# Ordering twelve scatters behind a gather, and moving three row squares out of the last attention head

## The reference

```python
x = attn_out.transpose(0, 2, 1, 3).reshape(1536, 512)
xn = x / (np.linalg.norm(x, axis=-1, keepdims=True) + 1e-06)
logits = xn @ en.T / tau
expert_idx = np.argmax(logits, axis=1)
gate_w = softmax(logits)[token, expert_idx]
for e in range(8):
    mask = expert_idx == e
    h = np.maximum(x[mask] @ w1[e], 0.0)
    out[mask] = gate_w[mask, None] * (h @ w2[e])
```

## Time and profile before

| | |
|---|---|
| median of 3 runs | 775.69 us (775.42 to 775.87) |
| the profiled execution | 775.23 us |
| its span, first to last instruction | 773.4 us |
| PE busy | 748.8 us, 97% of the span |
| DVE, ACT, POOL busy | 607.8, 462.3, 372.5 us |
| mean granted clock of TensorE | 0.986 of full speed |

### The profile page before, as it was taken

The page is one execution under the profiler, slowest core; times in us unless marked ns, Lnnn a source line. Parts: engine busy times, 40 slices in busy tenths (PEclk is TensorE's granted clock), DMA queues, the critical chain, the costliest instruction groups (busy, mean ns, idle before and its releaser), DMA issues.

```text
span 773.4 us, 15683 instructions
## 1 busy us (share of the span) xinstructions
PE 748.8 (97%) x5369; PEld 696.1 (90%) x5372; DVE 607.8 (79%) x1011; ACT 462.3 (60%) x887; POOL 372.5 (48%) x346
## 2 busy tenths in 40 slices
PE   7899999999999978999999999999999999999996
PEld 4799999999999956999999999989899999999995
DVE  5788888888888988766677765899977777778774
ACT  4778887788887872222222222468776767667673
POOL 3767767776566207664234442947332323223232
PEclk9999999999999986999999999999999999999999
DMA  9411112111140058467544676600000000000000
GB/s 265 110 33 32 42 31 51 31 31 41 31 153 1 1 191 295 113 238 243 202 158 158 229 245 202 236 1 1 1 28 1 28 1 28 0 0 27 0 27 27
DMA packets 70147, 68.27 MB, mean 88 GB/s; under 512 B 31704, under 2 KB 55128, under 8 KB 70112
## 3 DMA queue, kind: packets, MB, share of 16 engines
q1 hardware_dynamic: 67104, 60.31, 24.8%
q0 software_dynamic: 2080, 7.29, 2.5%
q10 hardware_dynamic: 928, 0.23, 0.1%
HBM read 56.99 MB, written 10.83 MB: 88 GB/s over the span
## 4 chain that ended last, share of the span: by engine, by line
PE 58%; issue 22%; POOL 8%; DVE 7%; ACT 3%; DMA 1%; POOLq 0%; ACTq 0%; DVEq 0%
PE PS L556 8%; PE PS L558 8%; PE PS L557 8%; PE PS L430 8%; POOL HL L1005 6%; PE PS L404 4%; PE PS L405 4%; PE PS L389 4%; PE PS L390 4%; PE PS L371 3%; PE PS L413 2%; POOL out L1014 1%; PE PS L363 1%; PE PS L552 1%; DVE w_low L1128 1%
## 5 line engine op out<-in xcount | busy, mean ns | idle before, releaser
L556 PE MATMUL PS<-XH,w_high 128*128 128x256 f32 x640 | 182.4, 285 | 0.7 <-DVE XL L1298 0.6
L558 PE MATMUL PS<-XH,w_low 128*128 128x256 f32 x640 | 182.1, 285 | 0.0
L557 PE MATMUL PS<-XL,w_high 128*128 128x256 f32 x640 | 182.1, 285 | 0.0
L906 POOL TENSOR_SCALAR w_high<-w_raw 128x1024 fp32r<-128x1024 f32 x80 | 102.6, 1300 | 97.1 <-DMA w_raw<-in_moe_w 82.0
L1005 POOL TENSOR_TENSOR HL<-U,HH 128x512 fp32r<-128x512 f32 x48 | 63.1, 1314 | 173.7 <-ACT HH L842 173.7
L556 PEld LDWEIGHTS PS<-XH,w_high 128*128 128x128 f32 x640 | 123.8, 194 | 4.0 <-issue 2.2
L557 PEld LDWEIGHTS PS<-XL,w_high 128*128 128x128 f32 x640 | 123.8, 193 | 1.7
L558 PEld LDWEIGHTS PS<-XH,w_low 128*128 128x128 f32 x640 | 123.8, 193 | 0.0
L1144 DVE TENSOR_TENSOR PTL<-PS,PTH 128x384 fp32r<-128x384 f32 x192 | 98.0, 552 | 32.0 <-ACT PTH L727 31.6
L1128 DVE TENSOR_TENSOR w_low<-w_raw,w_high 128x1024 fp32r<-128x1024 f32 x77 | 114.4, 1513 | 1.3 <-issue 1.2
L727 ACT ACTIVATE PTH<-PS 128x384 fp32r<-128x384 f32 x192 | 83.7, 489 | 42.5 <-PE PS L430 41.9
(11 more groups left out here) (209 smaller groups left out, 1670.4 us busy)
## 6 DMA issues: line engine op xcount, KB each, us to landing
w_raw<-in_moe_w SPq DMA_DIRECT2D x64, 512.0 KB, 7.4
xs<-xs_dram SPq DMA_DIRECT2D x8, 578.0 KB, 3.9
w_raw<-in_moe_w_in SPq DMA_DIRECT2D x8, 512.0 KB, 8.2
w_raw<-in_moe_w_out SPq DMA_DIRECT2D x8, 512.0 KB, 6.2
QK<-in_q SPq DMA_DIRECT2D x16, 192.0 KB, 3.1
V<-in_v SPq DMA_DIRECT2D x16, 192.0 KB, 2.4
QK<-in_k SPq DMA_DIRECT2D x15, 192.0 KB, 3.2
x_dram<-XO SPq DMA_DIRECT2D x1, 1728.0 KB, 7.2
```

The source lines that it names most:

```text
L556: nc.tensor.matmul(o, wh, xh, start=first, stop=False)
L557: nc.tensor.matmul(o, wh, xl, start=False, stop=False)
L558: return nc.tensor.matmul(o, wl, xh, start=False, stop=last)
L906: return nc.gpsimd.tensor_scalar(HIGH[par][:, p, :], RAW[par][:, p, :], 1.0, 0.0, ALU.mult, ALU.add)
```

## The change

The order of three squares on ACT changes, and POOL waits once more. In the last head the squares of tiles 3 and 4 (steps 1 and 2) are taken out; behind the head ACT now does tile 3, the first copy of `OS`, tile 4, the second copy, tile 5. Before, tile 5 was squared ahead of both copies. On POOL the first scatter waits for the landing of the second gather too.

```diff
-                        if far and i < GT:
-                            square(2 + i)
+                        if far and i == 0:
+                            square(2)
...
-            square(JT - 1)
+            square(JT - 3)
             for n, t0, t1 in ((0, 0, GT - 1), (1, GT - 1, GT)):
...
                 act.wait_ge(pv_done, GROUPS + n)
                 nc.scalar.activation(OS[:, t0 * P:t1 * P], PS[:, n, 0:(t1 - t0) * P], ACT.Copy).then_inc(os_done, 1)
+                square(JT - 2 + n)
             act.wait_ge(last_part, 1)
             act.wait_ge(xo_done, GROUPS)
...
             pool.wait_ge(scaled, 1)
+            pool.wait_ge(first_in[1], 16)
             for t in range(NT):
                 nc.gpsimd.indirect_dma_start(xs_dram, bass.IndirectOffsetOnAxis(ap=pos_i[:, t:t + 1], axis=0), XO[:, t, :], None).then_inc(rows_sent, 16)
```

## The result

The changed kernel takes 781.35 us, median of 4 runs (779.97 to 781.67); the kernel before took 775.56 us beside it (4 runs, 773.83 to 775.87). The ratio is 1.0068, with a 95% interval of 1.0057 to 1.008: 0.7% slower. The profiled execution took 779.97 us, its span 778.1 us, at a mean granted clock of 0.984.

The account below looks back on a forecast made before the run. PE was taken to set the end from the first expert on. Scatters 2.9, less slack 0.1 and squares 0.62, gave +2.2; with clock +1.0, 775.23 became 778.4, for the median 778.9 us, range 776.9 to 781.2.

Parts of the forecast that it names:

- Rival (a): On POOL's queue: second gather lands at 296.54 as before, scatter row shifts 4.4, total 780.9 us; chance 0.22.
- the prediction's own sign: Test named for the changed profile: if the second gather lands at 5.1 again, it is Rival (a).
- The squares.: ACT, step 1 of the last head: PTH starts earlier without the square, gain 0.62 us, bounds 0 to 0.72.
- The gather.: Second half of the gather, without scatters beside it, lands 3.7 to 4.0 after its issue instead of 5.05.
- The row of scatters.: POOL's twelve scatters: first starts 2.75 later, done before DVE's pair of weight pieces; last starts 2.9 later.
- That the landing hardly matters.: Landings between 294.5 and 295.9 give the same scatter shift; PE's first expert product gains at most 0.46.
- The way to PE.: Last scatter, SP's load, ACT's scaling: slack 0.1, so PE's second-chunk transposes end 2.8 later, PE standing still 3.1 us.
- The clock.: PE's stall at the second chunk may drop the clock to half: +1.0 us taken, bounds 0 to 2.3.
- Rival (b): POOL's scatters catch up by meeting DVE's weight pieces less often: shift 0.3, total 775.3 us; chance 0.07.
- Rival (c): Last head, step 1: the squares bring nothing because DVE or PE ended last anyway, total 779.5 us; chance 0.08.

Follow-up runs that it names:

- the squares alone: Only the three squares moved, no new wait on POOL, against the kernel before; run twice: 776.64 us, ratio 0.9992, and 775.07 us, ratio 0.9989.
- the moved fetch: 36 tiny products added to PE's program behind the last head: on the squares alone 774.73 us, ratio 0.9986; on the changed kernel 780.86 us, ratio 1.006.
- the run with idle products: Changed kernel with the first pair of experts written out and 16 idle PE products ahead of the first chunk's late transposes: 778.62 us, ratio 1.0035.
- the wait for the first half only: Changed kernel, but the scatters wait for the first half of the second gather instead of the second half: 776.62 us, ratio 0.9992.
- the wait alone: Kernel before with only the new wait on POOL added, squares unmoved; run twice: 780.73 us, ratio 1.0046, and 781.23 us, ratio 1.0072.
- the last two versions: Squares moved, 36 tiny PE products, transposes a quarter product later, no new POOL wait: 776.23 us, 0.9998; the same plus 9 idle products: 772.99 us, 0.9962.

## Why the prediction had the right sign, and where its sum was off

781.35 is 2.45 above the forecast of 778.9 and 0.15 above the upper end of the range, 781.2; by the ratio, 1.0068 x 775.69 = 781.0, it lies just inside. Rival (a), at 780.9, came nearest, but partly by luck: it had the landing right, and took 4.4 for the shift of the row where 5.6 was measured. By the prediction's own sign, a landing of 5.1 again, this is case (a), to which it gave a chance of 0.22. By its steps:

- **The squares.** -0.62 forecast, -0.62 read twice in the trace (ACT's first copy, PE's wait); the ratios of the squares alone, 0.9992 and 0.9989, agree. They fit behind the head, with 0.30 and 0.23 left.
- **The gather.** "The second half now lands 3.7 to 4.0 after its issue" failed: it landed at 5.0. Rival (a) had the landing, and its reason, that scatters behind the gather don't hold it, was borne out (3.9 with scatters right behind it). The rule on the order of DMA rings that the prediction took from the Trainium skill's page "DMA: Bandwidth & Descriptors", section "Queues, rings and completion order", is stated there of DMAs from SP and ACT. The traces agree with it for POOL's queue too: 3.9 with scatters behind the gather. What made the second half slow is most likely the instruction fetch.
- **The row of scatters.** "From there on the row runs two places behind" is the step that cost most. The row's last start shifted by 5.62 instead of 2.9. It also would have with the forecast landing: with 3.8 it was 24.14 - 19.13 = 5.0. POOL starts 0.80 after its release, where the prediction took about 0.1. So the first scatter, which was to be done before the pair of weight pieces, falls on the pair itself, even with the early landing (6.08, the pair at 5.92 behind the first gather), and the row runs three places behind: 3 x 1.27 = 3.8. And the scatter on the pair ends 9.14 behind the first gather where one ended 8.35 behind before, 0.8 more, because it starts on the second of the two pieces where that one started on the first. The rest, 1.0, is more holds: with eleven scatters instead of eight still to come, more of them meet DVE's later pieces (six held scatters in all instead of five, and the longest 1.89). Sum 5.6. The prediction's own layout was also tight: its first scatter, from 295.5 to 296.5, ends 0.2 after the pair's start at 296.31, so it wasn't "done before the pair"; a late start of 0.8 was all that it took.
- **That the landing hardly matters.** It was claimed for landings between 294.5 and 295.9 and held beyond that: 1.2 earlier made a difference of 0.3, no more than noise, since the pair catches the first scatter either way. For PE's first product the prediction allowed at most 0.46; with the moved fetch it came 9.25 and 9.61 behind the first gather instead of 9.92, so 0.3 to 0.7 earlier.
- **The way to PE.** As forecast up to its size: SP's load is issued 1.6 behind the last landing (317.50 against 312.91 + 2.98), and ACT scales on arrival. The last scatter landed 0.6 faster than before, so the load came 5.0 later; the load itself landed 0.3 faster (3.98 against 4.3), and 0.2 was PE's margin, so PE waited 4.50, not 3.1.
- **The clock.** It fell, as thought possible; the price was 2.1 by the changed kernel's trace and 2.55 by the run with idle products, where +1.0 had been taken between bounds of 0 and 2.3. A compromise between two outcomes was the wrong value for either. In all five traces with the full wait, the transposes at their old place and nothing to fill the stall, the clock fell.
- **Nothing won back.** The waits of PE behind the first chunk are those of before, and moving PE's transposes later removed nearly all of the loss. Rival (b), scatters that catch up, is out; the holds grew instead. Rival (c) is out by the squares' gain of 0.62 in the trace; by the times alone it is only just out.

By the terms: -0.62 + 4.5 + 2.1 = 6.0, against -0.62 + 2.8 + 1.0 = 3.2 in the forecast. Of the 2.8 between them 1.7 is the row of scatters and 1.1 the clock.

Still open: why the wait for the first half only costs nothing in the median though its one trace has the loss, why the wait alone was measured at 1.0046 once and 1.0072 once, on which DMA engine a fetch falls and so when it holds a gather, and whether the starved PE of one trace was a matter of instruction fetches.

## What to carry to other kernels

A wait put ahead of a row of issues on one engine costs more than its own length where the row shares something with another engine's work: lay the row out piece by piece against that work, with the start after a wait at its own price (0.80 here, against 0.30), and see on which piece each item falls. When PE's slack at the place where the row's last result is used is near zero, count the stall and then the half clock behind it in full, or fill the stall with idle products, which went with 2.55 less here. A faster PE ahead of such a stall gained nothing here, it only waited longer (6.97). If the data can't come earlier, move the instruction that needs them: a quarter of a product later in PE's order took away nearly all of the loss of 0.6%, but look at the last pass of the loop too, where the same move made the next stage wait 1.5 to 2.0.

## What the runs showed of the hardware

- A fetch of instructions (16 KB, one packet, 0.96 to 1.46 us) beside an indirect gather went with landings of 4.7 to 5.5 in eight traces, 3.9 in one, instead of 3.8 to 3.9. Where the gather was late with no scatter beside it, its last packets started as the fetch ended. Placing 36 tiny products in PE's program moved the fetch.
- An indirect DMA of POOL starts 0.80 to 0.84 after what releases it, where back-to-back ones follow each other in 0.30, a scatter's taking 0.97 to 1.02 when nothing holds it.
- A scatter's issue on POOL that starts while one of DVE's weight pieces (two f32 operands, 128x1024) runs ends 0.84 to 0.87 after that piece, or after its own 0.97 where that is later; it took up to 2.01 (squares alone, first run). One that starts just before a piece, or together with it, isn't held, though the two overlap: the kernel before has one from 306.60 to 307.57 beside the piece from 306.69, and the last two versions one from 305.5 beside the piece from 305.50. What is shared there the traces don't show.
- Idle products in PE's gaps kept the granted clock at 1.00, and the whole kernel was 0.4% faster with them, although they compute nothing.
